# Attention scores as one matmul per head in half of the array's rows, in place of one over a block-diagonal k

## What is computed

```python
k_p = k.reshape(B, H, 72, 8, 64).mean(axis=3)      # 576 keys pooled by 8 to 72
v_p = v.reshape(B, H, 72, 8, 64).mean(axis=3)
scores = q @ k_p.T / 8
attn = softmax(scores)
x = (attn @ v_p), heads side by side               # 4608 tokens x 512
x = relu(x @ w_in) ** 2 @ w_out
h = x @ w_in2
g = 0 where h <= -1, h where h >= 1, else (h + 1) ** 2 / 4
out = g @ w_out2
```

## Time and profile before

| | us |
|---|---|
| median of 3 runs | 1786.73 (1786.61 to 1787.14) |
| the profiled execution, its own time | 1784.99 |
| span of its trace (first to last instruction) | 1783.2 |
| PE busy | 1750.7 (98%) |
| PEld busy | 1412.3 (79%) |
| DVE busy | 761.4 (43%) |
| ACT busy | 551.2 (31%) |
| POOL busy | 235.8 (13%) |
| mean granted TensorE clock | 0.993 of full |

### The profile page before, as it was taken

One profiled execution on the slowest core, in us unless ns is written; L12 is line 12 of the kernel. 1 busy time (PEld: TensorE's weight loads), 2 busy tenths in 40 slices (PEclk: granted clock), 3 DMA queues, 4 the chain that ended last, 5 costly groups with the idle time before them and its releaser, 6 DMA issues.

```text
span 1783.2 us, 21965 instructions
## 1 busy us (share of the span) xinstructions
PE 1750.7 (98%) x8160; PEld 1412.3 (79%) x8160; DVE 761.4 (43%) x1208; ACT 551.2 (31%) x965; POOL 235.8 (13%) x264
## 2 busy tenths in 40 slices
PE   6899999999999999999999999999999999999999
PEld 4577778777777777778888788888888888888887
DVE  4564444434344443442235434343434343434343
ACT  3444333333333333332224322222222222222222
POOL 5342312313132232320000000000000000000000
PEclk8899999999999999999999999999999999999999
DMA  6454314242242322323025302020101020201000
GB/s 180 133 153 149 91 54 129 74 128 75 70 123 74 122 86 71 119 64 119 1 95 165 119 1 71 1 71 0 71 0 71 0 71 0 71 0 71 0 24 24
DMA packets 122436, 131.03 MB, mean 73 GB/s; under 512 B 44032, under 2 KB 76800, under 8 KB 122368
## 3 DMA queue, kind: packets, MB, share of 16 engines
q1 hardware_dynamic: 122368, 130.05, 23.3%
HBM read 82.84 MB, written 47.19 MB: 73 GB/s over the span
## 4 chain that ended last, share of the span: by engine, by line
PE 95%; DVE 2%; DMA 1%; ACT 1%; POOL 1%; issue 0%; SPq 0%; ACTq 0%; POOLq 0%
PE ps_h L715 44%; PE ps_y L737 44%; PE ps_a L657 2%; PE ps_a L684 2%; PE ps_a L700 2%; PE ps_a L672 1%; DVE sq_f L563 1%; DMA attn_out_hl<-xo_hl 1%; POOL kv_raw L392 0%; DVE probs L543 0%; DVE stat L541 0%; ACT act_f L462 0%; DMA kv_raw<-in_v 0%; DVE w_lo L532 0%; DMA xc<-attn_out_hl 0%
## 5 line engine op out<-in xcount | busy, mean ns | idle before, releaser
L715 PE MATMUL ps_h<-xc,w_hi 128*128 128x512 f32 x2304 | 721.4, 394 | 3.1 <-DMA xc<-attn_out_hl 2.1
L715 PEld LDWEIGHTS ps_h<-xc,w_hi 128*128 128x128 f32 x2304 | 426.5, 188 | 98.5 <-issue 11.7
L715 PE MATMUL ps_h<-xc,w_lo 128*128 128x512 f32 x1152 | 450.3, 391 | 0.0
L737 PE MATMUL ps_y<-w_hi,g_hl 128*128 128x512 f32 x1152 | 378.3, 389 | 3.1 <-DVE stage L587 2.2
L737 PE MATMUL ps_y<-g_hl,w_hi 128*128 128x512 f32 x1152 | 367.3, 400 | 2.6 <-DVE g_hl L567 2.6
L563 DVE TENSOR_TENSOR sq_f<-act_f 128x512 f32<-128x512 f32 x144 | 112.3, 780 | 421.5 <-ACT act_f L462 421.5
L737 PEld LDWEIGHTS ps_y<-g_hl,w_hi 128*128 128x128 f32 x1152 | 210.2, 188 | 58.6 <-issue 15.6
L737 PEld LDWEIGHTS ps_y<-w_hi,g_hl 128*128 128x128 f32 x1152 | 216.3, 188 | 49.0 <-DVE stage L587 2.6
L715 PEld LDWEIGHTS ps_h<-xc,w_lo 128*128 128x128 f32 x1152 | 216.5, 188 | 46.9
L469 ACT ACTIVATE act_f<-act_f,half_bias 128x512 f32<-128x512 f32 x144 | 104.1, 723 | 478.5 <-DVE act_f L574 478.5
L737 PE MATMUL ps_y<-g_hl,w_lo 128*128 128x512 f32 x576 | 226.5, 393 | 0.0
(11 more groups left out here) (52 smaller groups left out, 905.7 us busy)
## 6 DMA issues: line engine op xcount, KB each, us to landing
attn_out_hl<-xo_hl SPq DMA_DIRECT2D x64, 288.0 KB, 2.3
xc<-attn_out_hl SPq DMA_DIRECT2D x36, 512.0 KB, 3.9
mlp_out_hl<-stage SPq DMA_DIRECT2D x36, 512.0 KB, 4.3
xc<-mlp_out_hl SPq DMA_DIRECT2D x36, 512.0 KB, 5.9
kv_raw<-in_k SPq DMA_DIRECT2D x32, 288.0 KB
q_raw<-in_q SPq DMA_DIRECT2D x128, 72.0 KB, 2.0
kv_raw<-in_v SPq DMA_DIRECT2D x32, 288.0 KB
out<-stage SPq DMA_DIRECT2D x36, 256.0 KB, 2.1
```

Source lines behind the costliest of these rows:

```text
L715: mm = nc.tensor.matmul(ps_h[:, f % 2, :], left[:, f, kd * P:(kd + 1) * P], xc[:, buf, right, kd, :], start=(kd == 0 and n == 0), stop=(kd ...
L737: mm = nc.tensor.matmul(ps_y[:, m, :], left, right, start=(f == 0 and n == 0), stop=(f == NF - 1 and n == 2))
```

## The change

The block-diagonal tile goes. `k_t` (128 x 72) holds both heads' pooled k, one below the other, as the transpose leaves it, so that ACT copies it in one instruction and POOL has nothing to zero. Each 96 queries now take two matmuls in place of one: head 0 from partitions 0 to 63, head 1 from partitions 64 to 127, each with 64 rows, 96 stationary columns and 72 moving columns. The two heads' scores go to two banks: `ps_a` has the one in bank a and the other in bank b, and for odd units of batch 0 so does `ps_h`. Inside `probs` and `stat` the order of the six groups is now head, tile instead of tile, head.

Since the scores now use the bank that the transposes of q use, those transposes have a wait more: in later batches for `shifted` of unit 0 before those of unit 1, and in batch 0 for `shifted` of unit w - 2.

```diff
-        k_bd = sb("k_bd", [P, 2 * SP_])
+        k_t = sb("k_t", [P, SP_])
...
-        def score_bank(b, u):
-            return ps_h[:, 1, :] if first_batch(b) and u % 2 else bank_b
+        def score_banks(b, u):
+            return ps_h if first_batch(b) and u % 2 else ps_a
...
-            nc.gpsimd.memset(k_bd[:], 0.0).then_inc(zeroed, 1)
-            pool.wait_ge(zeroed, 3)
+            pool.wait_ge(zeroed, 2)
...
-                    for a in range(2):
-                        nc.scalar.copy(k_bd[a * D:(a + 1) * D, a * SP_:(a + 1) * SP_],
-                                       k_columns(b, w // 2)[a * D:(a + 1) * D, :]).then_inc(k_copied, 1)
+                    nc.scalar.copy(k_t[:], k_columns(b, w // 2)).then_inc(k_copied, 1)
...
-                    scores = groups(score_bank(b, u)[0:QT, 0:GRP * SP_])
-                    nc.vector.tensor_reduce(stat[:, u % 2, 0, :], scores, AX_X, ALU.max).then_inc(max_done, 1)
+                    scores = score_banks(b, u)[0:QT, :, 0:NJ * SP_].rearrange("p a (j n) -> p a j n", j=NJ)
+                    nc.vector.tensor_reduce(head_stat(u % 2, 0), scores, AX_X, ALU.max).then_inc(max_done, 1)
                     dve.wait_ge(max_done, b.times(NU, u + 1))
-                    nc.vector.tensor_tensor(groups(probs[:, u % 2, :]), scores, row_stat(u % 2, 0),
+                    nc.vector.tensor_tensor(by_head(probs[:, u % 2, :]), scores,
+                                            head_stat(u % 2, 0).unsqueeze(3).to_broadcast([QT, 2, NJ, SP_]),
                                             ALU.subtract).then_inc(shifted, 1)
...
                     for j in range(NJ):
-                        mm = nc.tensor.matmul(score_bank(b, u)[0:QT, j * 2 * SP_:(j + 1) * 2 * SP_],
-                                              q_t[:, j * QT:(j + 1) * QT], k_bd[:], start=True, stop=True)
+                        for a in range(2):
+                            mm = nc.tensor.matmul(score_banks(b, u)[0:QT, a, j * SP_:(j + 1) * SP_],
+                                                  q_t[a * D:(a + 1) * D, j * QT:(j + 1) * QT],
+                                                  k_t[a * D:(a + 1) * D, :], start=True, stop=True)
                     mm.then_inc(scores_ready, 1)
                 w = q_unit(b, s)
                 if w is not None:
 
                     if later:
                         pe.wait_ge(p_copied, b.times(NU, max(w - 1, 0)))
+                        if w == 1:
+                            pe.wait_ge(shifted, b.times(NU, 1))
+                    elif w >= 2:
+                        pe.wait_ge(shifted, w - 1)
```

More of the change, by code:

```diff
@@ L216, in groups, with by_head, head_stat @@
             return ap.rearrange("p (r n) -> p r n", r=GRP)
+        def by_head(ap):
+            return ap.rearrange("p (a j n) -> p a j n", a=2, j=NJ)
         def row_stat(par, i):
             return stat[:, par, i, :].unsqueeze(2).to_broadcast([QT, GRP, SP_])
+        def head_stat(par, i):
+            return stat[:, par, i, :].rearrange("p (a j) -> p a j", a=2)
         def chunk_slots(f, side):
@@ L648, in attention_slot @@
                     pe.wait_ge(q_copied, b.times(NU, u + 1))
-                    pe.wait_ge(k_copied, b.times(2 * KD, 2 * (u // 2 + 1)))
+                    pe.wait_ge(k_copied, b.times(KD, u // 2 + 1))
                     if u >= 2 and later:
@@ L700, in attention_slot @@
                             mm = nc.tensor.transpose(prob_banks(b)[0:SP_, a, j * QT:(j + 1) * QT],
-                                                     probs[:, w % 2, (2 * j + a) * SP_:(2 * j + a + 1) * SP_],
+                                                     probs[:, w % 2, (a * NJ + j) * SP_:(a * NJ + j + 1) * SP_],
                                                      ident[0:QT, 0:QT])
```

## The result

| | before | after |
|---|---|---|
| median of 9 runs, us | 1786.73 (1784.60 to 1788.86) | 1791.72 (1788.10 to 1794.39) |
| ratio | | 1.0028, 95% interval 1.0019 to 1.0037 |
| profiled execution, own time | 1784.99 | 1788.10 |
| span of its trace | 1783.2 | 1786.3 |

The forecast was 1792.5 us, slower. The change costs 5.0 us by the medians. The profile after is that of the fastest of its nine runs.

A forecast was written before the change was run, and what follows sets the result against it. The prediction took PE as the bound, busy 98% of the span. Later batches' +6.3 us and batch 0's -0.5 us gave +5.8 us on 1784.99, plus 1.74 us to the runs' median: 1792.5 us, range 1781 to 1806.

The forecast's parts named there:

- its sum of 5.8 us: Whole kernel: 6.3 us more in the seven later batches, less 0.5 us in batch 0.
- The block of scores: A later unit's scores on PE: 0.89 us in place of 0.74, 0.15 us more, pairs 0.09 us apart.
- the way in and out: Per block of scores on PE: entering and leaving the array's tiled mode costs 0.35 us, read from the product with v.
- The waits: PE's waits for DVE: unit 1 absorbs the 0.15 us; units 3, 5, 7 pay 0.10 each; unit 0 pays 0.15.
- A later batch: Each of seven later batches: 3 x 0.15 + 3 x 0.10 + 0.15 = 0.90 us more, 6.3 us in all.
- a sign of error: Wrong if the block is under 0.74 us, pairs are twelve steps, or later batches grow under 0.5 or over 1.5 us.
- Batch 0: At the start, lower clock: blocks 0.34 us shorter, -0.5 us in all (0 to -1), uncertainty 2 us both sides.
- this case alone: The prediction's main case for the whole kernel: 1792.5 us, 1788 to 1799 by itself, chance 0.50.
- row halves switch without a drain: Rival for the score blocks: mode changes free, block 0.57 us, 0.17 less; 1782 us, faster; chance 0.15.
- loads pair, streams don't: Rival for the score blocks: loads overlap but streams do not, 0.36 us more per block; 1803 us; chance 0.15.
- nothing pairs: Rival for the score blocks: loads and streams both one after the other, 0.69 us more per block; 1819 us; chance 0.08.
- It comes out even: Rival: way in and out about 0.2 us, or a start that gives back some us; 1787 us; chance 0.12.

The follow-up runs named there:

- Experiment 1: Changed kernel with each score matmul over all 128 rows (half of a block-diagonal k) instead of row halves; 1802.24 us, ratio 1.0090 to the kernel before.
- the two kernels without gaps: Changed kernel with 58 satisfied-wait instructions added on PE, at its very start (1787.91 us) or spread over chunk 0 (1787.38 us).
- The kernels with batch 0 alone: Tiled scores only in batch 0, later batches as before: unpadded 1785.68 us, 154 instructions spread over chunk 0 1785.83, 154 at the start 1789.85.
- experiment 10: Changed kernel with 29 satisfied-wait instructions spread over chunk 0, loop head at 1750; 1802.70 us, ratio 1.0091 to the kernel before.
- heads apart: Changed kernel with a unit's score matmuls reordered, head 0's three issued before head 1's three; 1800.66 us, ratio 1.0072 to the kernel before.
- experiment 2: Changed kernel with 58 satisfied-wait instructions added at PE's very start; 1787.91 us, ratio 1.0010 to the kernel before.
- experiment 3: Kernel before with 198 satisfied-wait instructions added on PE in three places, its loop head where the changed kernel has it; 1797.43 us, ratio 1.0067.

## Why the prediction was right, and where not

The time was right to 0.8 us, but that is partly luck: of its sum of 5.8 us about 3 us are not in the traces, and some 4 of the measured 5.0 us come with something that it didn't have.

- **The block of scores: right.** 0.86 us for 0.89; the start 0.32 us after the last MLP record, pairs under 0.02 us apart, 0.085 us for the 0.09 from pair to pair. Experiment 1 confirms the term that decided the sign: 0.32 us for the way in and out, where the prediction took 0.35 from the product with v. The page "TensorEngine Tiling (Array Packing)" of the Trainium skill says in "Key Properties" that changing the tiling mode drains TensorE, while tiles of one mode run independently. The rows of halves of rows agree, with 0.32 us for the way in and out and starts 0.006 us apart. The Trainium skill's page "TensorE: Matmul & The Clock Gate", "Measured speedup vs the span model", counts one matmul and about 4 ns per further tile. The 0.006 us within a pair agree; the block as a whole does not, since the rule has no price for the way in and out, and without one it would have been shorter than before.
- **The waits: right.** Unit 1's absorbed the longer block (0.57 left, 0.6 forecast), those of units 3, 5 and 7 went, unit 0's new one costs nothing, DVE kept 0.60 us.
- **A later batch: mis-sized.** "Per batch: ... 0.90 us, times 7 = 6.3 us" measured 0.42 to 0.50 in the two kernels without gaps and up to 0.56 in the changed kernel itself; 0.47 times 7 = 3.3. Most of these are below the 0.5 that the prediction named as a sign of error. Of the missing 0.4, 0.21 comes from the block (0.03 in seven units). Unit 1's wait shrank by 0.17, 0.05 more than its block grew. The rest, 0.1 to 0.2, is in the MLP records behind the blocks: before, nine to eleven of the 24 steps behind a block are 0.231 to 0.236 us in place of 0.227, after a tiled block six or seven. Summed over a chunk the excess fell from about 0.97 to 0.75 us. This was read from the two traces and not tested alone.
- **Batch 0: right in the trace, small in the time.** A block went from 1.52 to 1.17 us (8.68 to 10.20, and 8.84 to 10.01), -0.35 for the forecast -0.34. From the first transpose to unit 2's maximum it is 9.14 for 10.11 us. The kernels with batch 0 alone give -0.5 and -0.7 us for the forecast -0.5, within their noise.
- **The place of the loop: missed.** No step of the prediction spoke of it, and "For this case alone I would say 1788 to 1799" had no room for the 1802.7 us of experiment 10. The changed kernel with its loop out of the gaps is at 1787.4 to 1787.9 us, so some 4 of the 5.0 us go with the place and about 1 with the change (interval -0.7 to +2.3; the traces say 7 x 0.47 - 0.5 = +2.8, a little above it). The two profiles show 2.2 and 3.0 us of the 4 in gaps; the remainder is not located. What the prediction left out is PE's wait for its own code behind a jump back, which no row that it read could show: in the kernel before, issued work covers it.

The rivals: "row halves switch without a drain" falls with the 0.32 us, "loads pair, streams don't" and "nothing pairs" with the starts of the pairs. "It comes out even", with 0.12, is what the change does when the loop's place is taken out of the comparison, though not through a cheap way in and out. So the forecast slower came true for this program mostly by luck, for a reason that the prediction did not have.

## What to carry to other kernels

Small matmuls in tiles pay a way in and out per block: here six steps of 0.12 us became six of 0.085, which saves 0.21 us, against 0.32 for the way. The 0.085 us is near the 0.08 estimated for a 96-column load from the earlier trace rows, not the 0.06 of 72 streamed columns, and it is the same with full rows (experiment 1); no run varied the load's width. Issue the tiles of a pair alternately, because apart they lost half of their overlap here. Before a difference of some tenths of a per cent is put down to an edit, look for PE gaps that have no releaser right behind a long loop's jump back and for a packet of the instruction queue in them, and time the kernel again with some idle instructions ahead of the loop, placed where PE has work issued.

## What was not expected of the hardware

- A jump back of PE's first loop (2284 or 2484 records a turn) takes its sequencer 3.3 to 3.9 us, with a 16,384-byte packet of the instruction queue inside. It is hidden by work issued ahead. In the loop of 1579 records a turn it takes 0.21 to 0.24 us, without a packet, and a jump that is not taken 0.08 us.
- Behind the long jump a second stand of 3.1 to 5.0 us can follow, until the next block of code has landed. The code's place decides whether issued work covers it. With heads at 1523, 1625 and 1779 there is no gap, at 1721 gaps of 1.0 to 2.2 us, and at 1750 gaps of 5.0 us: 15.3 us of time between two kernels that differ in 29 idle instructions, three times what the change was timed at.
- The gaps of 1.0 to 1.8 us left the clock alone (the chunk is longer by the gap only). Those of 2.06 us with heads apart and 2.16 us in experiment 1 were each followed by seven MLP matmuls at the lower level, 1.5 or 1.6 us more, and the two of 5.0 us by about eleven.
- A satisfied wait costs PE's sequencer about 0.11 us: with 58 of them ahead of batch 0 the first transpose is at 7.96 us (experiment 2), with 90 at 11.54 (experiment 3). Spread over chunk 0 they cost nothing that shows.
